# Moving four weight sums of the second layer's first block from VectorE to GpSimd, and re-ordering three engines around it

## The reference

```python
# attention: 2 x 12 heads, 448 positions, head size 64
scores = cap * np.tanh(scale * np.matmul(q, k.transpose(0, 1, 3, 2)) / cap)
attn   = np.exp(scores - scores.max(-1)); attn /= attn.sum(-1) + 1e-9
x      = np.matmul(attn, v)                     # as 896 tokens x 768
# first layer: 768 -> 2048 -> 768
h = x @ w_in;   g = np.where(h > 0, h, np.exp(np.minimum(h, 0)) - 1);   x = g @ w_out
# second layer: 768 -> 2048 -> 768
h = x @ w2_in;  g = np.maximum(0.01 * h, h);                            y = g @ w2_out
```

## Time and profile before

| | |
|---|---|
| median of three runs | 575.18 us (574.24 to 575.58) |
| profiled execution | 574.8 us |
| its span | 573.0 us |
| TensorE (PE) busy | 557.3 us, 97% |
| VectorE (DVE) busy | 468.9 us, 82% |
| ScalarE (ACT) busy | 352.6 us, 62% |
| GpSimd (POOL) busy | 275.8 us, 48% |

### The profile page before, as it was taken

The page is one execution under the profiler, slowest core; times in us unless marked ns, Lnnn a source line. Parts: engine busy times, 40 slices in busy tenths (PEclk is TensorE's granted clock), DMA queues, the critical chain, the costliest instruction groups (busy, mean ns, idle before and its releaser), DMA issues.

```text
span 573.0 us, 8610 instructions
## 1 busy us (share of the span) xinstructions
PE 557.3 (97%) x2908; PEld 500.6 (87%) x2908; DVE 468.9 (82%) x758; ACT 352.6 (62%) x606; POOL 275.8 (48%) x273
## 2 busy tenths in 40 slices
PE   7999899999999999999999999989999999999997
PEld 5677789889998999999999999879999998999997
DVE  5899998878875133898988999889999779999881
ACT  6999998999995455654644454536454445544440
POOL 6789998799965655552000003857666520000000
PEclk9999999999999999999999999999999999999999
DMA  6466665445423233335644332031113225536251
GB/s 171 103 157 142 149 158 127 125 137 139 97 65 93 85 112 110 111 110 173 207 136 161 124 99 67 1 110 56 57 55 97 69 84 191 159 119 220 84 170 51
DMA packets 34172, 67.07 MB, mean 117 GB/s; under 512 B 6864, under 2 KB 18768, under 8 KB 34128
## 3 DMA queue, kind: packets, MB, share of 16 engines
q1 hardware_dynamic: 33984, 66.28, 40.4%
q10 hardware_dynamic: 144, 0.23, 0.1%
HBM read 63.70 MB, written 2.80 MB: 116 GB/s over the span
## 4 chain that ended last, share of the span: by engine, by line
PE 82%; DVE 10%; ACT 4%; issue 3%; DMA 1%; DVEq 0%; ACTq 0%
PE mlp_ps L1130 8%; PE mlp_ps L1132 8%; PE mlp_ps L1131 8%; PE o_ps L1130 6%; PE o_ps L1132 6%; PE o_ps L1131 6%; PE probs_t L1104 4%; PE scores L1130 4%; PE scores L1132 4%; PE scores L1131 4%; PE probs_t L1131 4%; PE probs_t L1132 4%; PE probs_t L1130 4%; PE scores L1089 3%; PE scores L1090 3%
## 5 line engine op out<-in xcount | busy, mean ns | idle before, releaser
L560 POOL TENSOR_TENSOR w_lo<-w_raw,w_hi 128x768 fp32r<-128x768 f32 (+1 forms) x62 | 104.3, 1682 | 62.1 <-ACT w_hi L622 61.7
L560 POOL TENSOR_TENSOR w_lo<-s_sum,w_hi 128x384 fp32r<-128x384 f32 x32 | 38.8, 1229 | 114.5 <-ACT w_hi L622 114.5
L622 ACT ACTIVATE w_hi<-s_sum 128x768 fp32r<-128x768 f32 (+1 forms) x64 | 43.4, 684 | 76.7 <-DVE s_sum L881 51.8
L622 ACT ACTIVATE w_hi<-w_raw 128x768 fp32r<-128x768 f32 (+1 forms) x77 | 56.5, 737 | 31.1 <-PE o_ps L1132 15.7
L602 ACT ACTIVATE soft<-soft,neg_max 112x448 f32<-112x448 f32 x96 | 63.8, 677 | 0.5 <-DVE soft L759 0.5
L759 DVE TENSOR_SCALAR_CACHE_REDUCE soft<-soft,neg_abs 112x448 f32<-112x448 f32 x96 | 60.8, 670 | 2.5 <-ACT soft L592 2.2
L1130 PE MATMUL mlp_ps<-x_hi,w_hi 128*128 128x448 f32 x132 | 49.1, 372 | 0.0
L766 DVE TENSOR_TENSOR p_lo<-probs_t,p_hi 112x896 fp32r<-112x896 f32 x37 | 40.3, 1090 | 10.7 <-ACT p_hi L611 10.6
L1132 PE MATMUL mlp_ps<-x_hi,w_lo 128*128 128x448 f32 x132 | 48.2, 366 | 0.0
L1131 PE MATMUL mlp_ps<-x_lo,w_hi 128*128 128x448 f32 x132 | 48.2, 365 | 0.0
L592 ACT ACTIVATE soft<-scores 112x896 f32<-112x896 f32 x47 | 43.7, 930 | 6.1 <-PE scores L1090 6.1
(11 more groups left out here) (238 smaller groups left out, 1749.7 us busy)
## 6 DMA issues: line engine op xcount, KB each, us to landing
w_raw<-w_units SPq DMA_DIRECT2D x120, 384.0 KB, 3.2
q_raw<-qT SPq DMA_DIRECT2D x24, 224.0 KB, 2.8
k_raw<-kT SPq DMA_DIRECT2D x23, 224.0 KB, 2.8
v_raw<-v_rows SPq DMA_DIRECT2D x24, 112.0 KB, 3.8
inv_all<-inv_rows SPq DMA_DIRECT2D x24, 112.0 KB, 3.1
y_t<-y_out SPq DMA_DIRECT2D x12, 224.0 KB, 2.8
inv_rows<-row_inv SPq DMA_DIRECT2D x24, 1.8 KB, 2.6
k_raw<-kT ACTq DMA_DIRECT2D x1, 224.0 KB, 3.4
```

Of the source, the lines that this page charges most:

```text
L560: pool.tensor_tensor(w_part(w_lo, n), w_source(n), f32(w_part(w_hi, n)), ALU.subtract).then_inc(w_lo_pool, 1)
L622: nc.scalar.activation(w_part(w_hi, n), w_source(n), ACT.Copy).then_inc(w_hi_done, 1)
```

## The change

Five edits:

- GpSimd forms block 0's four weight sums (`first_block_sum`), behind its own last split of `second(0)` and ahead of the split of block 0's first weight. They count on a semaphore of their own, `s_pool_done`. VectorE's list loses them.
- ScalarE takes the high part of p1's input (y11) ahead of block 0's first two weights, instead of behind them.
- ScalarE takes p2's input (y21) right behind eight weights of blocks 0 and 1, ahead of the loop over the blocks, instead of behind two more weights and the copy of (0,p1). The order of (0,p1)'s copy and the two weights in the loop stays.
- VectorE's list at the border gets a new order, with both differences of y ahead of block 1's sums, y21 ahead of p6's low part, and three of block 1's sums behind it. p2's low part stands ahead of the loop.
- In the attention, GpSimd's first three weight splits move from the end of steps 12, 16 and 20 to the end of steps 13, 17 and 21.

```diff
 SUM_ITEMS = ([n for n in range(GEMM1) if item_name(n)[1] in SUMS]
-             + [GEMM1 + BLOCK_AT[i, p] for i in range(HF) for p in SUMS]
+             + [GEMM1 + BLOCK_AT[i, p] for i in range(1, HF) for p in SUMS]
              + [n for n in range(GEMM2[1], ITEMS) if item_name(n)[1] in SUMS])
...
         def sum_done(n):
+            if item_name(n)[0] == "blocks" and item_name(n)[2] == 0:
+                return s_pool_done, SUMS.index(item_name(n)[1]) + 1
             return s_done, SUM_ITEMS.index(n) + 1
...
+            def first_block_sum(p):
+                n = GEMM1 + BLOCK_AT[0, p]
+                raws = ITEM_RAWS[n]
+                for r in raws:
+                    pool.wait_ge(*loaded(r))
+                pool.wait_ge(*split_done(GEMM1 - 9))
...
+                pool.tensor_tensor(dst, *args).then_inc(s_pool_done, 1)
...
-                if s in (12, 16, 20):
-                    split_w((s - 12) // 4)
+                if s in (13, 17, 21):
+                    split_w((s - 13) // 4)
             for n in LO_ON_POOL[units_ending_at(STEPS - 1)[0] + AHEAD:]:
+                if n == GEMM1:
+                    for p in SUMS:
+                        first_block_sum(p)
                 split_w(n)
...
             second(0)
+            x_high("p1")
             w_high(GEMM1)
             w_high(GEMM1 + 1)
-            x_high("p1")
...
             w_high(GEMM1 + 7)
+            x_high("p2")
...
-                if i == 0 and p == "p1":
-                    x_high("p2")
...
             second(0)
-            for p in SUMS:
-                weight_sum(GEMM1 + BLOCK_AT[0, p])
-
-            weight_sum(GEMM1 + BLOCK_AT[1, "p5"])
-            weight_sum(GEMM1 + BLOCK_AT[1, "p6"])
             x_low("p1")
             dve.wait_ge(xc_split, X_GROUPS.index("p1") + 1)
             x_sum(y12, y12, y11, ALU.subtract)
-            weight_sum(GEMM1 + BLOCK_AT[1, "p3"])
+            x_sum(y11, y22, y11, ALU.add)
+
+            weight_sum(GEMM1 + BLOCK_AT[1, "p5"])
             x_low("p5")
-            x_sum(y11, y22, y11, ALU.add)
-            weight_sum(GEMM1 + BLOCK_AT[1, "p7"])
-            x_low("p6")
             dve.wait_ge(u3_done, HC)
             add_to(0, "p4", y21, kept_u2[0], y21_done)
+            x_low("p6")
+            weight_sum(GEMM1 + BLOCK_AT[1, "p6"])
+            weight_sum(GEMM1 + BLOCK_AT[1, "p3"])
+            weight_sum(GEMM1 + BLOCK_AT[1, "p7"])
+            x_low("p2")
```

More of the change, by code:

```diff
@@ L316, in build @@
         relu_done, act_done, g_done = sem("relu_done"), sem("act_done"), sem("g_done")
-        s_done = sem("s_done")
+        s_done, s_pool_done = sem("s_done"), sem("s_pool_done")
         t1_done, t2_done, t3_done, t4_done = (sem(f"t{i}_done") for i in range(1, 5))
@@ L560, in split_w @@
                 pool.tensor_tensor(w_part(w_lo, n), w_source(n), f32(w_part(w_hi, n)), ALU.subtract).then_inc(w_lo_pool, 1)
+            def first_block_sum(p):
[4 more added lines that the diff above has]
+                pool.wait_ge(*split_done(GEMM1 - 9))
+                dst, (lo, hi) = w_source(n), (slice(0, HALF), slice(HALF, UNIT))
+                if p == "p6" or p == "p3":
+                    ahead = GEMM1 + BLOCK_AT[0, SUMS[SUMS.index(p) - 1]]
+                    pool.wait_ge(*sum_done(ahead))
+                    before = w_source(ahead)
+                a11, a12 = w_raw[:, raws[0] % RAW, lo], w_raw[:, raws[0] % RAW, hi]
+                if p == "p5":
+                    args = a11, a12, ALU.add
+                elif p == "p7":
+                    args = a11, w_raw[:, raws[1] % RAW, lo], ALU.subtract
+                elif p == "p6":
+                    args = before, a11, ALU.subtract
+                else:
+                    args = a12, before, ALU.subtract
+                pool.tensor_tensor(dst, *args).then_inc(s_pool_done, 1)
             pool.memset(zero[:, :], 0.0).then_inc(zero_set, 1)
@@ L1018, in _ @@
             x_sum(y12, y12, y11, ALU.subtract)
-            weight_sum(GEMM1 + BLOCK_AT[1, "p3"])
+            x_sum(y11, y22, y11, ALU.add)
+            weight_sum(GEMM1 + BLOCK_AT[1, "p5"])
             x_low("p5")
-            x_sum(y11, y22, y11, ALU.add)
-            weight_sum(GEMM1 + BLOCK_AT[1, "p7"])
-            x_low("p6")
             dve.wait_ge(u3_done, HC)
             add_to(0, "p4", y21, kept_u2[0], y21_done)
+            x_low("p6")
[3 more added lines that the diff above has]
+            x_low("p2")
             for q in range(GEMM1 + 1, GEMM2[1] + 1):
                 i, p = BLOCK_SEQ[q - GEMM1 - 1]
-                if i == 0 and p == "p6":
-                    x_low("p2")
                 if p == "p6":
```

## The result

| | before | changed |
|---|---|---|
| median | 574.91 us (574.24 to 575.58, 4 runs) | **569.55 us** (569.11 to 571.38, 4 runs) |
| ratio | | 0.9918, interval 0.9902 to 0.9934 |
| profiled execution, its span | 574.8, 573.0 us | 571.38, 569.6 us |
| PE, VectorE, GpSimd busy | 557.3, 468.9, 275.8 us | 558.3, 467.6, 285.8 us |

A second set of six runs, on a chip where the kernel before took 574.22, gave 0.9928 (0.9914 to 0.9942). The page's line of busy time, which answers the earlier trace rows, says nothing of where the gain is: TensorE is busy for longer, in a shorter span, and GpSimd has 10 us more for four sums.

What follows compares the result with a forecast made beforehand. TensorE, busy for 97% of the span, was taken as the bound, so only its waits and matmul distance could give time. 1.1 + 2.4 + 1.7 = 5.2 us off 574.8 gave 569.6, as median 570.0; range 569.0 to 573.3.

Steps and rivals of the forecast that it cites:

- Attention: Attention: v splits of steps 13 and 17 come 1.83 us earlier, shortening TensorE's two waits; -1.1 us (0 to -1.4).
- Border: Border: with four sums on GpSimd and new orders, TensorE's three breaks go or shrink; -2.4 us (0 to -2.4).
- the three breaks: Border: TensorE's waits at (0,p6), (1,p3) and (0,p4), all hanging on VectorE; booked at -0.43, -1.47 and -0.53 us.
- The contention: Border: VectorE and GpSimd slow each other at SBUF; 1.8 us taken for the sums' meetings, up to 3.3 by the rule.
- Distance: Stage 4: without a border break TensorE keeps 0.2026 us per matmul instead of 0.2064; -1.7 us.
- Rival 1: Waits go, but the slow matmul distance stays, in stage 4 or later; 571.7 us, chance 0.28.
- Rival 3: GpSimd becomes the border's bound, losing 2.5 us over five products; 574.2 to 575.2 us; chance 0.12, shared with otherwise eaten gains.
- Rival 4: Slower: TensorE resumes from the attention's last wait in the slow distance; 577.3 us, chance 0.07.

Runs made afterwards that it cites:

- e3: Changed kernel with block 0's four sums back on VectorE, directly behind `second(0)`, all else of the change kept; 569.35 us, ratio 0.9915.
- e4: Kernel before with block 0's four sums moved to GpSimd as the only edit; 575.16 us, ratio 1.002.
- e5: e3 with ScalarE's old border order: p1's input behind two weights, p2's back in the block loop; 573.24 us, ratio 0.9984.
- e9: e3 with only one of ScalarE's two moves: p1's input ahead of the weights, p2's back in the loop; 572.70 us, ratio 0.9969.
- e10: e3 with only the other ScalarE move: p2's input ahead of the loop, p1's back behind two weights; 571.09 us, ratio 0.9939.
- e2: Changed kernel with the attention edit undone (weight splits at steps 12, 16, 20 again); 571.82 us, ratio 0.9949.
- e11: e3 repeated word for word, on one chip with e12; 569.82 us, ratio 0.9924.
- e12: Changed kernel repeated, on one chip with e11; 570.46 us, ratio 0.9928.
- e1: Kernel before with only the attention edit (GpSimd's first three weight splits at steps 13, 17, 21); 572.24 us, ratio 0.9971.
- e7: e3 with one more TensorE wait ahead of product p3 in each of blocks 2 to 7; 590.39 us.
- e8: e3 with VectorE's last split ahead of the second stage moved ahead of the last block's last maximum; 570.21 us, ratio 0.9913.
- e6: e3 with VectorE's border order put back to the old one, ScalarE's new order kept; 570.84 us, ratio 0.9923.

## Why the prediction was right, step by step

- **Attention**, -1.1: right in mechanism, too small by 0.3 us. The remaining wait was put at 0.3 to 0.5 and is 0.30. The term was mis-sized because I took ScalarE's loss from the "idle before" of two rows, 0.33 + 0.78. Its loss is the distance of two tanh starts less the usual 2.90. The timeline of before around the two waits:

```profile
48.67 0.95 ACT L592 ACTIVATE soft<-scores 112x896 f32<-112x896 f32 x1
...
52.07 0.92 ACT L592 ACTIVATE soft<-scores 112x896 f32<-112x896 f32 x1
...
60.79 0.93 ACT L592 ACTIVATE soft<-scores 112x896 f32<-112x896 f32 x1
...
64.61 0.91 ACT L592 ACTIVATE soft<-scores 112x896 f32<-112x896 f32 x1
```

  3.40 and 3.82 in place of 2.90: 0.50 + 0.92 = 1.42, and 1.36 and 1.4 were measured.
- **Border**, -2.4: the three breaks are gone, also the third, which I had called open. My times were in the clock of the trace before, so 0.82 us must be added to those of the changed kernel. The sums' end on GpSimd is then 353.3 against 352.5. I let VectorE leave `second(0)` at 352.9, it left at 352.4; p6's low part ends at 366.15 against 366.4 to 367.1, and p2's at 370.9, inside 370.4 to 371.6. So charging nearly every instruction as contended was too much by up to a microsecond at p6 and by nothing at p2. The third break had little margin: the low part for (0,p4) was done 0.55 us ahead of it, 0.40 more than where TensorE waits.
- **Attribution.** The prediction booked the four sums, 2.2 us, as what VectorE gains, and ScalarE's move of p1 only as a cost of 1.2 us. e3 and e4 show that the sums gave 0.26 us and nothing in time, e5, e9 and e10 that the moves on ScalarE are needed for all of it. The total came out although the work was given to the wrong part of the change, because the walk through VectorE's list took p1's and p2's high parts as early as the new order has them; to that extent it was luck. The contention was booked at 1.8 us; 2.05 was measured. The Trainium skill, "SBUF — State Buffer", section "Who interferes with whom", was weighed against the move: by the rows its rule is right in kind (1.08 becomes 1.90), and its price here stayed just below the 2.31 us saved, where up to 3.3 were reckoned.
- **Distance**, -1.7: right in size for stage 4, 1.75, and in kind for the changed kernel, e2, e3, e11 and e12. Rival 1 foresaw that it could come back at a later break, and in the profiled run it did, for 1.6 us behind 488; in the median it did not decide. That the same break can leave either distance is now shown (e4 and e5 against e1 and e9); the reading that the slow distance begins when TensorE resumes and lasts until the next break was that of one execution. e7 and e8 show that it can begin without a break, e6 that it can end without one. So the absence of breaks does not secure the 1.7 us: by e7 this term was in part luck.
- **Rival 3**, GpSimd as the bound: its splits did not get late for TensorE, which waits for nothing from 344 to 469 us. Rival 4 did not occur: from 178 to 360 us the distance is 0.2027 in all fourteen profiles.

## What to carry to other kernels

Where several engines work through fixed lists, look at what stands *ahead* of the wanted instruction in each list, and at whether that waits for something later: moving ready work ahead of waiting work on ScalarE was worth 1.4 us by the medians with VectorE's old order (e6 against e1) and 3.9 with its new one (e3 against e5). Moving 2.3 us of work from VectorE to GpSimd gave nothing, since VectorE paid 2.05 of it back in longer instructions and TensorE did not need the rest. Orders of two engines have to be tried together: VectorE's alone costs 1.0 us, ScalarE's alone gives 1.4, both give 2.9. And size a loss from the distance of starts of a repeated instruction, not from the idle field.

## What the hardware showed

- 448-column matmuls in a gapless run start 0.2027 or 0.2067 us apart at the same granted clock of 1.00. They held 0.2027 for up to 1443 matmuls (changed) and 0.2067 for up to 467 (e4), and changed at a break as short as 0.44 us and, in e6, e7 and e8, at none. Over the blocks and `second(1)` together, some 900 matmuls, that would be up to 3.6 us, which is about the spread of the kernel before, 572.6 to 576.4 us. The kernels without breaks at the border spread less, but not always: e3 and e11 run from 569.2 to 570.7, the changed kernel and e12 from 569.1 to 572.1.
- Four 128 x 384 sums take 2.31 us on VectorE and, beside VectorE, 8.2 on GpSimd. A VectorE instruction with both inputs in SBUF is 0.4 to 0.8 us longer beside GpSimd, and where it is the full 0.82, that doesn't depend on its size: 0.55 becomes 1.37 (128x384), 1.08 becomes 1.90 (128x896), 1.55 becomes 2.37 (128x1344). A GpSimd split of 128x384 takes 1.01 us beside VectorE's adds from PSUM and 2.33 beside its instructions on SBUF.
- After TensorE had stood still for 3.96 and 3.26 us the granted clock was 0.50 for the next 13 and 8 matmuls; after 1.74, 1.86 and 1.46 us it stayed 1.00. After 1.85 us it fell too, but only 1.5 us later, for 9 matmuls.
